# The second expert's first matrix loaded during the last group, and twelve narrow products one place later

## What is computed

```python
def reference(...):
    x = attention(q, k, v, g_norm)      # 8 x 8 heads x 576 x 64, linear, RMS-normalised
    x = _moe_ref(x, w_in, w_out)        # x: 4608 x 512;  relu(x @ w_in)**2 @ w_out, d_ff = 2048
    return _moe2_ref(x, ...)            # 8 experts, each token goes to one

def _moe2_ref(x, modality_id, w_gate, modality_bias, w1, w2):
    logits = x @ w_gate + modality_bias[modality_id]
    e_idx = np.argmax(logits, axis=1)
    ...
    for e in range(E):
        mask = e_idx == e
        h = np.maximum(x[mask] @ w1[e], 0.0)          # 512 -> 1024
        out[mask] = gate_w[mask, None] * (h @ w2[e])  # 1024 -> 512
```

## Time and profile before

| | us |
|---|---|
| median of three runs | 1400.74 |
| lowest, highest | 1399.47, 1401.35 |
| the profiled execution, its own time | 1399.94 |
| its span, first to last instruction | 1398.2 |
| PE busy in the span | 1368.1 |
| DVE, ACT, POOL busy | 793.6, 592.4, 500.6 |
| mean granted clock of PE | 0.994 |

### The profile page before, as it was taken

How to read it: one execution, slowest core, us unless ns; L and a number is a source line. 1 busy time by engine, 2 the same in 40 slices (tenths; PEclk the granted TensorE clock), 3 DMA queues, 4 the chain that set the end, 5 groups by cost and what they waited for, 6 DMA issues and landing times. The chain is left out here.

```text
span 1398.2 us, 20708 instructions
## 1 busy us (share of the span) xinstructions
PE 1368.1 (98%) x6935; PEld 1114.7 (80%) x6935; DVE 793.6 (57%) x1677; ACT 592.4 (42%) x1201; POOL 500.6 (36%) x589
## 2 busy tenths in 40 slices
PE   4999999999999999999999999999999999999997
PEld 3888788888887887887888887877788788888876
DVE  2556575574574564574674665546565555555555
ACT  2444333334334243333343343334555555555553
POOL 2633232232132132132232234504555555555551
PEclk9999999999999999999999999999999999999999
DMA  9635546656656556566464464778995113851270
GB/s 223 174 94 166 178 138 186 190 122 189 192 130 198 178 125 210 169 135 215 157 151 143 151 153 150 198 268 208 327 375 189 47 47 114 301 202 47 68 263 20
DMA packets 184037, 237.45 MB, mean 170 GB/s; under 512 B 58862, under 2 KB 102286, under 8 KB 183954
## 3 DMA queue, kind: packets, MB, share of 16 engines
q1 hardware_dynamic: 169650, 214.85, 51.2%
q0 software_dynamic: 9472, 19.96, 4.4%
q10 hardware_dynamic: 4832, 1.57, 0.6%
HBM read 148.07 MB, written 89.30 MB: 170 GB/s over the span
## 5 line engine op out<-in xcount | busy, mean ns | idle before, releaser
L668 POOL TENSOR_TENSOR stage<-stage,stage_hi 128x512 f32<-128x512 f32 x128 | 170.9, 1336 | 552.7 <-ACT stage_hi L1147 552.6
L1483 DVE TENSOR_TENSOR g_sb<-g_sb 128x512 f32<-128x512 f32 x144 | 101.5, 705 | 321.9 <-ACT g_hi L1211 314.2
L1209 ACT ACTIVATE g_sb<-ps_h 128x512 f32<-128x512 f32 x144 | 86.1, 598 | 458.2 <-PE ps_h L815 259.5
L813 PE MATMUL ps_y<-g_hi,weights 128*128 128x512 f32 x576 | 231.0, 401 | 0.0
L813 PE MATMUL ps_h<-xT_hi,weights 128*128 128x512 f32 (+1 forms) x580 | 230.5, 397 | 0.0
L815 PE MATMUL ps_h<-xT_hi,weights 128*128 128x512 f32 (+1 forms) x580 | 225.6, 389 | 0.0
L814 PE MATMUL ps_h<-xT_lo,weights 128*128 128x512 f32 (+1 forms) x580 | 225.3, 388 | 0.0
L815 PE MATMUL ps_y<-g_hi,weights 128*128 128x512 f32 x576 | 224.9, 390 | 0.0
L814 PE MATMUL ps_y<-g_lo,weights 128*128 128x512 f32 x576 | 224.5, 390 | 0.0
L1237 ACT ACTIVATE kv_sb<-ps_h 32x256 f32<-32x256 f32 x456 | 170.9, 375 | 120.0 <-PE ps_h L999 114.6
L999 PE MATMUL ps_y<-weights,xT_hi 128*128 128x512 f32 x656 | 177.0, 392 | 0.9 <-DVE xT_lo L1664 0.5
(11 more groups left out here) (267 smaller groups left out, 1747.8 us busy)
## 6 DMA issues: line engine op xcount, KB each, us to landing
stage<-in_moe_w SPq DMA_DIRECT2D x128, 256.0 KB
w_hi<-stage_hi SPq DMA_DIRECT2D x128, 256.0 KB
w_lo<-stage SPq DMA_DIRECT2D x128, 256.0 KB
weights<-w_hi SPq DMA_DIRECT2D x32, 1024.0 KB, 5.7
weights<-w_lo SPq DMA_DIRECT2D x32, 1024.0 KB, 6.6
rows<-y_sb SPq DMA_DIRECT2D x36, 256.0 KB
q_sb<-in_q SPq DMA_DIRECT2D x28, 256.0 KB, 3.1
k_sb<-in_k SPq DMA_DIRECT2D x30, 160.0 KB, 3.4
```

The source lines that it names most:

```text
L668: pool.tensor_tensor(stage[n % 2][:, :], stage[n % 2][:, :], stage_hi[n % 2][:, :].bitcast(F32), ALU.subtract).then_inc(split_lo, 1)
L813: pe.matmul(out_ap, lhs[0], rhs[0], start=start, stop=False)
L1209: act.activation(g_sb[:, :], ps_h[c % 2][:, 0:GROUP], ACT.Relu).then_inc(h_read, 1)
L1483: dve.tensor_tensor(g_sb[:, :], g_sb[:, :], g_sb[:, :], ALU.mult).then_inc(g_done, 1)
```

## The change

The second expert's pieces 0 to 3 move into group 8: `FIRST_WEIGHTS_AT` now begins at chunk 5 and holds pairs (expert, piece); a piece of expert 1 waits until the chunks of `w_out` that lay there have been used. The loads after the group are gone. The slot products, with their wait on `slots_done`, move from the end of hidden(1) to behind the first quarter of output(0), and the four products of `ps_next` from there to the middle of output(0). DVE, ACT and POOL run the same instructions in the same order as before.

```diff
                     if m.c == GROUPS - 1:
-                        for piece in FIRST_WEIGHTS_AT.get(c, ()):
-                            sp.wait_ge(h_ps, m.count(CH, 2 * piece + 2))
-                            load_weights(0, 0, piece)
+                        for e, piece in FIRST_WEIGHTS_AT.get(c, ()):
+                            sp.wait_ge(h_ps, m.count(CH, 2 * piece + (2 if e == 0 else 5)))
+                            load_weights(e, e, piece)
...
-            FIRST_WEIGHTS_AT = {8: (0,), 9: (1,), 10: (2,), 11: (3,), 12: (4,), 13: (5,), 15: (6, 7)}
+            FIRST_WEIGHTS_AT = {5: [(0, 0)], 6: [(0, 1)], 7: [(0, 2)], 8: [(0, 3)], 9: [(1, 0)], 10: [(0, 4)], 11: [(1, 1)],
+                                12: [(0, 5), (1, 2)], 13: [(1, 3)], 14: [(0, 6)], 15: [(0, 7)]}
...
             sp.wait_ge(y_ps, GROUPS)
-            load_w1(1, range(2))
             for T in range(EARLY):
                 sp.wait_ge(early_row_in[T], 64)
             store_rows(Group(GROUPS - 1))
-            load_w1(1, range(2, 4))
...
             sp.wait_ge(lists_in, 16)
-            load_w2(1)
+            for piece in range(4, 8):
+                sp.wait_ge(weights_in[1][piece - 2], filled(1))
+                load_weights(1, 1, piece)
...
                     pe.matmul(ps_b[0:1, 0:E], ones[:, 0:1], before[:, 0, :], start=True, stop=True).then_inc(counts_ps, 1)
+
+            def third_places(place):
+
+                if place == "quarter of output":
                     pe.wait_ge(slots_done, TILES + 1)
                     for b in range(SLOT_BLOCKS):
                         for t in range(TILES):
                             last = pe.matmul(ps_slot_ids[:, b:b + 1], ...)
                     last.then_inc(slot_ids_ps, 1)
-
-            def third_places(place):
-
-                if place == "quarter of output":
+                elif place == "middle":
                     pe.wait_ge(ids_in_block_done, 2)
```

More of the change, by code:

```diff
@@ L574, in _, with load_w1 @@
             all_groups(group)
[L576 to L581, removed]
+            def load_w1(e):
+                sp.wait_ge(h_ps, tile_before(sp, e - 1) * 2 + (GROUPS * CH + 2))
+                sp.sem_inc(passed, 1)
+                for piece in range(4):
                     at_once = 2
@@ L584, in load_w1 @@
                         sp.wait_ge(weights_in[e % 2][piece - at_once], filled(e))
-                    elif e > 1:
+                    else:
                         sp.wait_ge(weights_in[(e - 1) % 2][piece + 6], filled(e - 1))
@@ L589, in load_w2 @@
             def load_w2(e):
-                if e > 1:
-                    sp.wait_ge(y_ps, tile_before(sp, e - 1) + (GROUPS + 1))
-                    sp.sem_inc(passed, 1)
+                sp.wait_ge(y_ps, tile_before(sp, e - 1) + (GROUPS + 1))
+                sp.sem_inc(passed, 1)
                 for piece in range(4, 8):
```

## The result

The change makes the kernel slower: 1407.07 us (median of 14 runs, 1404.38 to 1411.26) against 1400.73 (14 runs), a ratio of 1.0043 with a 95% interval of 1.0033 to 1.0052. That is 6.3 us, where +1.7 was forecast. The profiled execution took 1407.36 us, with a span of 1405.6.

The account below looks back on a forecast made before the run. PE, busy 98% of the span, was taken as the bound. Terms 2.2 + 1.0 - 1.5 = +1.7 us on the profiled 1399.94 gave 1401.6; with the runs' median 0.8 above, 1402.4 us was predicted, range 1398.2 to 1405.8.

Parts of the forecast that it names:

- Slot products moved behind a quarter: +2.2 us: Counts to hidden(2): PE idles 3.5 us for DVE in place of 1.35, then runs partly at 1.2 GHz; +2.2 us.
- second case (+1.7): Counts to hidden(2): 1.2 GHz for the same 6.8 us as before, 949.0 to 955.8; +1.7 us.
- third (+2.8): Counts to hidden(2): 1.2 GHz until the slot products are done; +2.8 us.
- fourth case (+4.2): Counts to hidden(2): 1.2 GHz through the second quarter of output(0) too; +4.2 us.
- slower rival: Behind the counts: clock stays at 1.2 GHz through the second quarter; 1405.2 us, chance 0.23.
- Tile 3's rows: +1.0: Ahead of tile 3: later next_set makes POOL start its fetch some 2.5 us later; +1.0 us, bounds 0 and 2.3.
- Weights earlier: -1.5: Ahead of tile 4: earlier weights leave its fetch empty queues, removing the 1.55 us idle time; -1.5 us.
- No more comes of it: Beyond tile 4's idle time: where PE is full, earlier weights move nothing.
- In the last group: 0: Chunks 5 to 7: added loads run beside pieces of the splits and PE stays full; 0 us.
- collision rival: Loads in chunks 5 to 9 delay the stage pieces, PE idles some 4 us; 1406 us, chance 0.04.
- faster rival: At the joint the clock survives (-0.9), tile 3 in time, tile 4 -1.55; 1398.3 us, chance 0.08.
- the one without effect: At the joint the wait for DVE is shorter than read, all terms near 0; 1400.7 us, chance 0.08.

Follow-up runs that it names:

- e1: The kernel before with the slot products and the products of ps_next moved as in the change, loads left where they were; ratio 1.0031.
- e4: The change's kernel with the slot products one quarter later still, behind the second quarter of output(0); ratio 1.0027.
- e9: The change's kernel with the first quarter of hidden(2) spread between the slot products, one big product behind every two; ratio 1.0046.
- e3: The change's kernel with 15 extra unused big products between the counts and the first quarter of output(0); ratio 1.0004.
- e10: The change's kernel with half of hidden(2), twelve big products, moved behind the counts; ratio 1.0010.
- e2: The change's kernel with the slot products back at the end of hidden(1), so only the loads are moved; ratio 0.9986.
- e8: e7 with the moved loads of the change; ratio 0.9993.
- e7: The kernel before with hidden(2)'s first quarter between counts and slot products, and its second quarter spread between the slot products; ratio 0.9984.
- e5: The kernel before with the first quarter of hidden(2) moved between the counts and the slot products; ratio 0.9996.
- e6: e5 with the moved loads of the change; ratio 0.9991.
- e12: e6 with SP waiting for tile 3's rows before the last two pieces of the second expert's second matrix; ratio 0.9986.
- e11: e8 with SP waiting for tile 3's rows before it loads the second expert's second matrix; ratio 0.9999.

## Why the prediction was wrong

**The term that failed is "Slot products moved behind a quarter: +2.2 us".** Its certain part held: an idle time of 3.5 us was forecast, 3.51 measured. The clock part failed. I took the low period from the one in the trace, 6.8 us, and put the term between its second case (+1.7) and its third (+2.8). Measured is 4.67 us (4.85 in e1), above even the fourth case (+4.2), because the first products of the third quarter were slow too. What came was beyond the slower rival, to which I gave 0.23.

By the profile the terms sum to +5.8 us, and the forecast had +1.7. Of the 4.1 us between them 2.5 are this term, 1.2 are small waits that the forecast put at nothing (ahead of tiles 5 and 6, and behind tile 3), and 0.5 are tile 3.

Why 6.8 us was not to be carried over can be seen in the rows now. In the kernel before, the clock fell behind 1.35 us of idle time and some slot products, and the rest of the slot products were over at 952.58: it rose after 3.2 us of big products in a row. In the change it fell earlier relative to the work, in the idle time; 2.7 us of big products came and did not lift it; then 5 us of slot products; and it rose 4.5 us into the next big ones. In all these traces the clock rose only behind a stretch of big products, so narrow products that come first put the rise off, and a length counted from the fall can't be carried to another order. e4 shows it by experiment: the same idle time, the big products together, and the period is 6.8 us. What sets the moment of the rise is open. It came 2.2 us into the big products in e9, 3.2 before and 4.5 in the change; in e4 5.3 us of them were over and the slot products had just begun. And 2.7 us of them, the first quarter, did not bring it in the change. The mechanism of the rival is supported by e3 and e10 as well, in which filled time brings back 4.1 us (17.97 - 13.87) and 8.3 us (20.7 - 12.4) of the segment; of the 8.3, 3.0 are idle time that became work (3.51 to 0.54) and the rest is clock.

The Trainium skill's rule, that the throttled state is the default and only activity lifts it ("TensorE: Matmul & The Clock Gate", Part 1), stood in the text as +2.8 against my +2.2. The runs agree with its sense: in the change the clock stayed at 0.50 for 13.7 us, through the slot products, and rose only in big products. It was the better guide, though +2.8 was short too. That the point varies from run to run agrees with the twelve runs of e2, one and the same kernel, whose mean clocks lie between 0.994 and 0.997.

**Tile 3's rows: +1.0** was +1.46, and that it came so near is luck. `next_set` came at 964.0, 4.1 us after the slot products, as worked out. But POOL began at 965.39, 1.4 us behind it, which the forecast left out. Counted from the counts this is 4.5 us later than before (16.9 against 12.3), where I had 2.5, and what hid it is that PE was 4.7 us late and not 2.2. The last fetch, its issue ended at 973.2, was used at 977.90, 4.7 us later. The profile of the change:

```profile
965.39 0.32 POOL L783 CAST y_sb<-v_sb 128x8 int32<-128x8 f32 x2 [11.77 <-issue]
...
972.22 0.95 POOL L740 DMA_INDIRECT k_sb<-rows,v_sb  x1 [0.30 <-issue]
```

```profile
977.90 0.45 DVE L1367 STREAM_TRANSPOSE k_sb<-k_sb 128x256 f32<-128x256 f32 x1 [1.89 <-DMA k_sb<-rows,v_sb]
```

The row stores did land sooner without weights beside them, but only by some 1.4 us, as e8 shows; in the change `next_set` was later than they.

**Weights earlier: -1.5** holds as a size (the 1.55 us ahead of tile 4 are gone), but not wholly as a cause: in e1 they go without the moved loads. The lists were issued at 960.65, 12.1 us behind the counts; the forecast was 957.4, 10.8 behind them. "No more comes of it" was wrong: tiles 5 and 6 wait 0.70 and 0.33 us now, and 0.54 and 0.35 in e2. Slower fetches are not the reason. Tile 5's last rows were used 4.7 us after their last issue in the change (995.7 to 1000.36) and 5.4 us before (987.5 to 992.89), both beside weights. These are DVE's rows before, in the change and in e2:

```profile
992.89 0.45 DVE L1367 STREAM_TRANSPOSE k_sb<-k_sb 128x256 f32<-128x256 f32 x1 [1.92 <-DMA k_sb<-rows,v_sb]
```

```profile
1000.36 0.45 DVE L1367 STREAM_TRANSPOSE k_sb<-k_sb 128x256 f32<-128x256 f32 x1 [1.69 <-DMA k_sb<-rows,v_sb]
```

```profile
992.78 0.45 DVE L1366 STREAM_TRANSPOSE k_sb<-k_sb 128x256 f32<-128x256 f32 x1 [1.86 <-DMA k_sb<-rows,v_sb]
```

In e2 the rows come when they came before, and PE, without its wait for tile 4, is 1 us earlier (995.4 against 996.38). In the change they come 7.5 us later than before, and PE only 6.5 (1002.84): POOL began this fetch 8.2 us later (990.27 against 982.07), because it first waited for DVE's copy of an output (985.39, before 977.18), which stands in DVE's order behind tile 3's late rows. So part of what tile 4 gains is lost again two tiles later. That e2 is 2 us faster nevertheless shows that the loads alone were a gain.

**In the last group: 0** held. In e2, e3, e4 and e9, which all have the early loads, PE is without idle time there. The collision rival, the faster rival and the one without effect did not come.

Of the signs named beforehand, the idle time behind the counts, a clock of 0.50 for 6.8 us or more and the vanished idle time ahead of tile 4 were there; the profile names "issue" and not `xT_lo` as what ended the idle time, but DVE wrote `xT_lo` until 952.1, just before, and e4's row of the same wait names it. The lists were 0.7 us later than the sign said, counted from the counts. None of the signs of being wrong came: they watched for a clock that does not fall, and not for one that stays down longer.

What stays open: how much of the difference between e7 (0.9984) and e8 (0.9993), or e5 and e6, is real; their intervals overlap. e2, e7 and e12 are faster than before by about 0.15%, and none of the kernels is faster than e2 beyond its interval.

## What to carry to other kernels

Before moving narrow products off a place where PE waits for another engine, ask what they covered there: the wait that appears costs its own length and then, as here, a low clock over what follows. The low clock lasted here until big products had run in a row again, so narrow products behind the wait lengthened it. Fill such a gap with big products that are due anyway; here that took 4.4 us off the segment, of which some 2 us at most reached the kernel's time. Then look at once for the next wait behind it, because a PE that is early only pays if lists, rows and weights are early too, and here they were not.

## What was not expected of the hardware

- Twelve one-column products in a row, 2.6 us without any idle time on PE, were followed by a fall to 1.2 GHz in e3's profiled execution (954.7 to 958.1), and not in e5's, where the same run stood behind other big products.
- A fall at the joint cost 3.4 us at half clock (e3, e4), 6.8 us (before, e2, e4) or 13.7 us (the change, e9).
- Twelve narrow and six big products in alternation kept the full clock when they met it (e7, e8), and did not bring it back when it was low (e9).
- Gathering the last rows of a tile took 1.7 us from the end of the issue to their use with quiet queues (e11), and 3.9 to 4.7 us beside loads of 1 MB (e8, the change).
- The same kernel does not get the same clock each time: e11's twelve runs had mean granted clocks from 0.993 to 0.998, and the one with 0.998 was the fastest.
